# Scores of the two-headed tile moved ahead of the second head's transposes, and two copies exchanged between ScalarE and VectorE

## Chip, core and metric

The kernel runs on one core of a Trainium2 chip. The metric is the time of one execution on the device in microseconds (us); lower is better. The engines are TensorE (PE in the profile; PEld is its loading of weights), VectorE (DVE), ScalarE (ACT), GpSimd (POOL) and SyncE (SP), which issues most of the transfers.

## What is computed

Three stages in float32. The change touches only the first, the attention:

```python
def _attn_ref(q, k, v):                     # q, k, v: (4, 8, 1152, 64)
    B, H, S, D = q.shape
    scale = 1.0 / np.sqrt(D)
    q_pool = q.reshape(B, H, S // 2, 2, D).mean(axis=3)
    scores = scale * np.matmul(q_pool, k.transpose(0, 1, 3, 2))
    scores = scores - np.max(scores, axis=-1, keepdims=True)
    attn = np.exp(scores)
    attn = attn / (np.sum(attn, axis=-1, keepdims=True) + 1e-09)
    return np.matmul(attn, v)
```

The attention's output, as 2304 rows of 512, goes through a soft mixture of 8 experts (gating with `moe_phi`, two matrices of each expert) and then through `g = h - tanh(h)`, `g @ w_out`.

## The kernel before

**Pairs and rounds.** The 32 heads are done as 16 pairs. Each pair's 576 pooled queries are four tiles of 128 for each head and a rest of 64; the rests of both heads make one tile of 128 rows. So a pair has five rounds: r = 0, 1 (tiles 0 and 1, two heads each), r = 2, called MIX (one tile that holds 64 rows of either head), r = 3, 4 (tiles 2 and 3). Pairs 0, 1, 14 and 15 are written out, the other twelve run in a loop of two.

**A round.** TensorE multiplies q by K (`scores`, lines 256 and 259; q and K are held as a high and a low part, so three products) in three chunks of 512, 512 and 128 columns, into PSUM banks 0, 1, 2 for head 0 and 3, 4, 5 for head 1; MIX needs only banks 0 to 2. VectorE takes the row extreme: two reductions over the first chunks (L398), then one over the short chunk and both results (L402); for head 1 in one instruction over all 1152 columns (L410). ScalarE does the exponential of each head (L493, 1152 columns). TensorE transposes the nine 128x128 blocks of each head's probabilities (`turn_prob`, L290): head 0's chunks back into banks 0, 1, 2, head 1's into 6, 5, 4; for MIX in the order 2, 0, 1 into banks 0, 2, 1. They are copied to SBUF (`evac`): chunk 0 of both heads and chunk 1 of head 1 by ScalarE (L466), the others by VectorE (L372, for MIX L370). The product with V (`pv`, L306, bank 7) of what earlier rounds left is put between the scores and the transposes of rounds 3, 4, 0 and 1; MIX has none.

**The next pair's K and q.** In round MIX, TensorE also transposes the next pair's K (nine blocks, L239, banks 3 to 5, called `k_row`) and q (a rest block L247, then four blocks L242, bank 6 and the end of bank 5, `q_row`). VectorE copies K to `k_raw` (L448), ScalarE copies q to `q_raw` (L515), and GpSimd splits both into high and low parts (lines 208 to 214) for the next pair's round 0.

**What sets the order.** Everything is written out by hand: each engine runs its own list in program order and waits on semaphores. `first_evac` counts copied chunks 0, `second_a` and `second_b` chunk 1 of head 0 and of head 1, `third_evac` chunks 2. `banks_free` holds the waits of the scores for the banks. `first_evac`, `second_b` and `q_sum` are waited for ahead of the next pair's transposes, `k_copied` and `q_evac` ahead of round 3's scores, which overwrite `k_row` and `q_row`. The attention's output of the pair before is transposed (`turn_out`, L314 and L316) and scaled by VectorE (L427, L432) in rounds 1 and 3; `empty_v` (ScalarE) copies the V product out of bank 7.

After the last pair come the gating and the experts. The weights of experts 1 to 3 are loaded when marks in the last pair are reached, those of expert 4 when the gating ends, the later ones as slots come free.

Of the kernel before, what the change touches and what calls it, by code (L numbers as in the profile page):

```python
# [10 lines left out]
P = 128  # L11
# [6 lines left out]
def attention(nc, dram, sizes, sb, x, ident, rep, rep_ready, rep_step, early, prefetch):  # L18
# [38 lines left out]
    PV_EVAC_AT = {0: 0, 2: 1}  # L57

    with ExitStack() as ctx:
# [169 lines left out]
        def turned_as(r, c):  # L229

            return (1, 2, 0)[c] if r == MIX else c

        @block.tensor
        def _(pe):
            def turn_k_and_q(n, q_dst):

                pe.wait_ge(k_in, n * 32 + 32)
                for m in range(KT):
                    last = nc.tensor.transpose(k_row[:, m * P:(m + 1) * P], k_nat[:, m].rearrange("p h d -> p (h d)"), ident[:])  # L239
                last.then_inc(ktr_full, 1)  # L240
# [22 lines left out]
            def banks_free(p, r, c, first, last):  # L263

                before = tiles_of(p, r)
                if c == 0:
                    if r == MIX + 1:
                        wait(pe, third_evac, before)
                        if not last:
                            pe.wait_ge(k_copied, p + 1)  # L270
                    else:
                        wait(pe, first_evac, before - 1)
# [3 lines left out]
                elif r == MIX + 1:  # L276
                    wait(pe, first_evac, before)
                    if not last:
                        pe.wait_ge(q_evac, p + 1)
                elif r != MIX:  # L280
                    wait(pe, second_b, doubles_of(p, r))

            def turn_prob(p, r, h):
# [3 lines left out]
                for c in (2, 0, 1) if r == MIX else range(NCH):  # L287
# [32 lines left out]
            pe.wait_ge(ident_ready, 1)  # L320
            turn_q_rest(0, ps[:, TBANK, BANK - P:BANK])
            turn_k_and_q(0, first_q_row)

            def body(p, par, first, last):
                for r in range(ROUNDS):
                    for c in range(NCH):
                        banks_free(p, r, c, first, last)
                        if r == 0 and c == 0:
                            if first:
                                pe.wait_ge(first_kl, 1)  # L330
                                pe.wait_ge(first_ql, 1)
                            wait(pe, k_low, p)
                            wait(pe, q_low, p)
                        scores(p, par, r, c)

                    wait(pe, first_evac, tiles_of(p, r))
                    if r == MIX and not last:
                        wait(pe, second_b, doubles_of(p, r))
                        turn_q_rest(p + 1, ps[:, TBANK - 1, BANK - P:BANK])
                        turn_k_and_q(p + 1, q_row)  # L340
# [3 lines left out]
                    turn_prob(p, r, 0)  # L344
                    if r != MIX:
# [3 lines left out]
                if last:  # L349
# [4 lines left out]
                    turn_out(p, 1)  # L354

# [26 lines left out]
        def _(dve):  # L382
# [52 lines left out]
            def body(p, par, first, last):  # L435
                for r in range(ROUNDS):
                    tau = tiles_of(p, r)
                    minimum_by_chunks(p, r)
                    if r != MIX:
                        minimum_of_row(p, r)  # L440
# [4 lines left out]
                    if r == MIX and not last:  # L445
# [4 lines left out]
                    for c in (2, 1) if r == MIX else (1, 2):  # L450
                        dve.wait_ge(ptr_full, tau * NCH + turned_as(r, c) + 1)
# [12 lines left out]
        def _(act):  # L464
# [35 lines left out]
            def body(p, par, first, last):  # L500
                for r in range(ROUNDS):
                    tau = tiles_of(p, r)
                    if r in PV_EVAC_AT and not first:
                        empty_v(p - 1, PV_EVAC_AT[r])
# [3 lines left out]
                    act.wait_ge(ptr_full, tau * NCH + turned_as(r, 0) + 1)  # L508
                    evac(copy, r, 0, 0).then_inc(first_evac, 1)
                    if r == MIX:  # L510
                        if not last:
                            act.wait_ge(qtr_full, p + 2)
                            act.wait_ge(k_copied, p + 1)
                            wait(act, q_low, p)
                            nc.scalar.activation(q_raw[:], q_row, ACT.Copy, scale=EXP_SCALE).then_inc(q_evac, 1)  # L515
                    else:
                        act.wait_ge(ptr_full, tau * NCH + NCH + 1)
                        evac(copy, r, 1, 0).then_inc(first_evac, 1)
# [727 lines left out]
```

## Time and profile before

| | before |
|---|---|
| median of 3 runs | 886.7 us (885.58 to 887.46) |
| the profiled execution | 885.63 us, its span 883.8 us |
| mean granted TensorE clock | 0.984 of full |
| TensorE busy (PE / weight loads) | 811.5 us (92%) / 597.8 us (68%) |
| VectorE / ScalarE / GpSimd busy | 531.0 (60%) / 483.5 (55%) / 248.6 us (28%) |

The span of the profiled execution lies 1.8 us under its own time, and that time 1.1 us under the median. In the rows, times are microseconds from the span's start. A row such as "[0.68 <-ACT prob L493]" says how long the engine sat idle before it, and what released it. A matmul's row on PE has a modelled end, so starts are the safer reading.

### The profile page before, as it was taken

Reading aid. Unit: us, or ns where it says so; the run is one execution under the profiler, and the core shown is the slowest. Engines: PE = TensorE matmul, PEld = TensorE weight load, DVE = VectorE, ACT = ScalarE, POOL = GpSimd, SP = SyncE. Lnnn points to the kernel's source line nnn. Section 1 sums busy time; section 2 is a strip of 40 time slices with the busy share of each in tenths; the row PEclk is TensorE's granted clock in tenths of the full one; section 3 lists DMA queues with packets and bytes.
Section 4 is the critical chain, followed back from the end, with each engine's and each line's share of the span. In section 5 each row is a group of like instructions: output and inputs, shape, how many; then the busy total and the mean of one; then the engine's idle time right before and its main releaser. Section 6 shows DMA issues by size and latency. Waiting matters only on the chain. (4 is left out here: it accounts for less than half of the span.)

```text
span 883.8 us, 16411 instructions
## 1 busy us (share of the span) xinstructions
PE 811.5 (92%) x5819; PEld 597.8 (68%) x5819; DVE 531.0 (60%) x984; ACT 483.5 (55%) x729; POOL 248.6 (28%) x154
## 2 busy tenths in 40 slices
PE   3899999999999999999999988878678999999998
PEld 3676776776667677676677665634236888888886
DVE  2666666666666766766766754430037667677663
ACT  2566566566566566566566554220048666766672
POOL 2304304404404403403403300000038344334432
PEclk9999999999999999999999999979889999999999
DMA  5353303303303303303303164348960000000000
GB/s 134 131 145 81 81 2 82 80 1 80 80 0 80 80 0 80 80 0 80 80 0 80 63 252 162 125 170 315 404 253 1 25 24 24 24 24 24 24 24 24
DMA packets 82160, 75.49 MB, mean 85 GB/s; under 512 B 42448, under 2 KB 60880, under 8 KB 81616
## 3 DMA queue, kind: packets, MB, share of 16 engines
q1 hardware_dynamic: 79792, 74.47, 26.5%
q10 hardware_dynamic: 2336, 0.59, 0.3%
q8 instruction: 21, 0.34, 0.2%
q14 instruction: 11, 0.09, 0.0%
HBM read 70.32 MB, written 4.72 MB: 85 GB/s over the span
## 5 line engine op out<-in xcount | busy, mean ns | idle before, releaser
L493 ACT ACTIVATE prob<-ps,neg_max 128x1152 f32<-128x1152 f32 x144 | 175.7, 1221 | 186.6 <-DVE spare L402 186.6
L290 PE MATMUL ps<-ident,prob 128*128 128x128 f32 x1296 | 169.7, 280 | 29.3 <-ACT prob L493 27.1
L290 PEld LDWEIGHTS ps<-ident,prob 128*128 128x128 f32 x1296 | 140.7, 142 | 72.5 <-ACT prob L493 63.9
L306 PE MATMUL ps<-probT,v_nat 128*64 128x256 f32 (+1 forms) x1152 | 153.6, 411 | 0.0
L398 DVE TENSOR_REDUCE part_neg<-ps 128x1 f32<-128x512 f32 x160 | 109.7, 692 | 45.7 <-PE ps L259 38.2
L372 DVE COPY probT<-ps 128x128 f32<-128x128 f32 (+1 forms) x192 | 75.5, 421 | 99.5 <-PE ps L290 99.5
L466 ACT ACTIVATE probT<-ps 128x512 f32<-128x512 f32 x208 | 117.1, 594 | 32.1 <-PE ps L290 32.0
L208 POOL TENSOR_TENSOR kT<-k_raw,ones 128x1152 fp32r<-128x1152 f32 x15 | 31.6, 2107 | 311.0 <-DVE k_raw L448 311.0
L259 PE MATMUL ps<-kT,qT_hi 64*128 64x512 f32 (+1 forms) x768 | 112.2, 369 | 2.6 <-DVE qT_lo L389 2.6
L306 PEld LDWEIGHTS ps<-probT,v_nat 128*64 128x64 f32 x1152 | 77.3, 136 | 52.2 <-issue 5.7
L963 PE MATMUL ps<-w_hi,g_even 128*128 128x512 f32 x320 | 102.6, 392 | 2.2 <-POOL g_even L1047 2.0
L259 PEld LDWEIGHTS ps<-kT,qT_hi 64*128 64x128 f32 x768 | 68.1, 188 | 28.1 <-issue 10.6
L410 DVE TENSOR_SCALAR_CACHE_REDUCE spare<-ps 128x1152 f32<-128x1152 f32 x64 | 86.5, 1352 | 0.0
L963 PE MATMUL ps<-w_hi,g_odd 128*128 128x512 f32 x256 | 81.7, 390 | 0.0
L1021 ACT ACTIVATE slot<-ps 128x1024 f32<-128x1024 f32 x36 | 37.0, 1028 | 64.7 <-PE ps L947 64.6
L963 PEld LDWEIGHTS ps<-w_hi,g_even 128*128 128x128 f32 x320 | 60.1, 188 | 15.7 <-POOL g_even L1047 3.0
L259 PE MATMUL ps<-kT,qT_lo 64*128 64x512 f32 (+1 forms) x384 | 69.4, 355 | 0.0
L1086 DVE SCALAR_TENSOR_TENSOR slot<-slot,ps 128x1024 f32<-128x1024 f32 x36 | 44.0, 1222 | 38.6 <-ACT ps L1023 38.6
L1047 POOL TENSOR_TENSOR g_even<-slot,g_even 128x1024 fp32r<-128x1024 f32 x20 | 48.2, 2409 | 58.1 <-ACT g_even L1008 58.1
L1093 DVE COPY_PREDICATED slot<-slot,ps 128x1024 f32<-128x1024 uint32 x36 | 49.3, 1370 | 22.0 <-DVE slot L1086 20.3
L963 PE MATMUL ps<-w_lo,g_even 128*128 128x512 f32 x160 | 62.5, 391 | 0.0
L963 PEld LDWEIGHTS ps<-w_hi,g_odd 128*128 128x128 f32 x256 | 48.1, 188 | 9.7
(144 smaller groups left out, 1038.5 us busy)
## 6 DMA issues: line engine op xcount, KB each, us to landing
slot<-in_moe_w SPq DMA_DIRECT2D x16, 2048.0 KB, 12.8
v_nat<-in_v SPq DMA_DIRECT2D x16, 576.0 KB, 5.0
k_nat<-in_k SPq DMA_DIRECT2D x30, 288.0 KB, 4.0
q_nat<-in_q SPq DMA_DIRECT2D x32, 256.0 KB, 4.1
out<-res SPq DMA_DIRECT2D x18, 256.0 KB, 2.0
slot<-in_moe_w_in SPq DMA_DIRECT2D x2, 2048.0 KB, 20.8
slot<-in_moe_w_out SPq DMA_DIRECT2D x8, 512.0 KB, 16.7
q_nat_r<-in_q SPq DMA_DIRECT2D x32, 32.0 KB, 3.5
```

The costliest lines, as they stand in the source:

```text
L259: last = nc.tensor.matmul(ps[:, 3 * h + c, 0:k1 - k0], q[par][HALF[h], at], kT[par][HALF[h], part, k0:k1], start=(n == 0), stop=(n == 2))
L290: last = nc.tensor.transpose(dst[:, n * P:(n + 1) * P], prob[h][:, kt * P:(kt + 1) * P], ident[:])
L306: last = nc.tensor.matmul(ps[64 * h:64 * h + D, VBANK, 0:n], v_nat[par][:, h, kt, :], probT[g][:, kt, h, :], start=(kt == 0), stop=(kt == ...
L372: return copy(probT[g][:, k0:k1, h, col:col + P], src.rearrange("p (c q) -> p c q", c=n))
L398: nc.vector.tensor_reduce(part_neg[:, c:c + 1], ps[:, c, :], AX.X, ALU.min).then_inc(part_done, 1)
L410: nc.vector.tensor_scalar(spare[1][:], flat[:, 3 * BANK:3 * BANK + S], LARGE, LARGE, ALU.min, ALU.min, accum_out=neg_max[:, j:j + 1]).then ...
L466: return nc.scalar.activation(dst, src, ACT.Copy)
L493: nc.scalar.activation(prob[h][:], row, ACT.Exp, bias=neg_max[:, j:j + 1], scale=-1.0, accum_out=sums).then_inc(exp_done, 1)
L963: last = nc.tensor.matmul(ps[:, 2 * HB + i, :], a[par][:, ft * CW + i * P:ft * CW + (i + 1) * P], w(ft), start=(ft == 0 and k == 0), stop= ...
L1047: nc.gpsimd.tensor_tensor(g_block(g_lo, par, b), g[b % 2], g_block(g_hi, par, b).bitcast(F32), ALU.subtract).then_inc(gl_done, 1)
L1086: nc.vector.scalar_tensor_tensor(tv[b % 2], sq[b % 2], 1.0, h_of(b), ALU.subtract, ALU.mult).then_inc(series_done, 1)
L1093: nc.vector.copy_predicated(tv[b % 2], big[b % 2].bitcast(mybir.dt.uint32), th).then_inc(tanh_done, 1)
```

## The change

Five edits. (1) TensorE: MIX's scores are issued between round 1's transposes of head 0 and those of head 1. To free their banks in time, head 0 of round 1 is transposed in MIX's order and places (chunk 2 into bank 0, chunk 0 into bank 2, chunk 1 into bank 1). (2) TensorE: the next pair's K is transposed chunk by chunk, each chunk behind the wait for its bank, with q's rest between and q's other blocks last. (3) VectorE: MIX's reductions come between the copies of round 1's two heads; VectorE takes chunk 1 of head 1 of that round. (4) ScalarE: it copies K (and then q) right after MIX's exponential and ahead of MIX's chunk 0; `empty_v` of the second group moves to round 1, between its two copies. (5) At the start, K is transposed ahead of q's rest.

```diff
-    PV_EVAC_AT = {0: 0, 2: 1}
+    SHORT_FIRST = ((MIX - 1, 0), (MIX, 0))
...
-            place = (2, 1, 0) if r == MIX else ((0, 1, 2), (TBANK, 5, 4))[h]
+            place = (2, 1, 0) if (r, h) in SHORT_FIRST else ((0, 1, 2), (TBANK, 5, 4))[h]
...
+            def turn_next_k_and_q(p):
+
+                pe.wait_ge(k_in, (p + 1) * 32 + 32)
+                turn_k(0)
+                wait(pe, third_evac, tiles_of(p, MIX))
+                turn_k(1)
+                wait(pe, second_b, doubles_of(p, MIX))
+                turn_q_rest(p + 1, ps[:, TBANK - 1, BANK - P:BANK])
+                turn_k(2)
+                wait(pe, first_evac, tiles_of(p, MIX))
+                turn_q(q_row)
...
+                if r == MIX:
+                    if c == 0:
+                        pe.wait_ge(third_evac, before - 1)
+                    elif c == 1:
+                        pe.wait_ge(second_a, p * ROUNDS + r)
+                    else:
+                        pe.wait_ge(first_evac, before - 1)
...
+            pe.wait_ge(k_in, 32)
+            for c in range(NCH):
+                turn_k(c)
             turn_q_rest(0, ps[:, TBANK, BANK - P:BANK])
-            turn_k_and_q(0, first_q_row)
+            turn_q(first_q_row)
...
                     turn_prob(p, r, 0)
+                    if r == MIX - 1:
+                        all_scores(p, par, MIX, first, last)
                     if r != MIX:
...
-                    if r == MIX and not last:
-                        dve.wait_ge(ktr_full, p + 2)
-                        wait(dve, k_low, p)
-                        nc.vector.tensor_copy(k_raw[:], k_row).then_inc(k_copied, 1)
                     group_free(dve, p, r)
...
+                    if r == MIX - 1:
+                        minimum_by_chunks(p, MIX)
                     if r != MIX:
                         dve.wait_ge(ptr_full, tau * NCH + NCH + 3)
                         evac(nc.vector.tensor_copy, r, 1, 2).then_inc(third_evac, 1)
+                    if r == MIX - 1:
+                        dve.wait_ge(ptr_full, tau * NCH + NCH + 2)
+                        evac(nc.vector.tensor_copy, r, 1, 1).then_inc(second_b, 1)
...
+                    if r == MIX and not last:
+                        act.wait_ge(ktr_full, p + 2)
+                        wait(act, k_low, p)
+                        copy(k_raw[:], k_row).then_inc(k_copied, 1)
+                        act.wait_ge(qtr_full, p + 2)
+                        wait(act, q_low, p)
+                        nc.scalar.activation(q_raw[:], q_row, ACT.Copy, scale=EXP_SCALE).then_inc(q_evac, 1)
                     group_free(act, p, r)
...
                     evac(copy, r, 0, 0).then_inc(first_evac, 1)
...
+                    if r == MIX - 1 and not first:
+                        empty_v(p - 1, 1)
```

TensorE, pair 1, from the transposes of round 1's head 0 (`prob_79`; head 1 is `prob_80`) to MIX's; before:

```order
L290 MATMUL ps<-ident,prob_79 128x128 x9
L290 MATMUL ps<-ident,prob_80 128x128 x9
L256 MATMUL ps<-kT_74,qT_hi_76 128x512 x2
L256 MATMUL ps<-kT_74,qT_lo_78 128x512
L256 MATMUL ps<-kT_74,qT_hi_76 128x512 x2
L256 MATMUL ps<-kT_74,qT_lo_78 128x512
L256 MATMUL ps<-kT_74,qT_hi_76 128x128 x2
L256 MATMUL ps<-kT_74,qT_lo_78 128x128
L247 MATMUL ps<-ident,q_both_r 128x128
L239 MATMUL ps<-ident,k_nat 128x128 x9
L242 MATMUL ps<-ident,q_both 128x128 x4
L290 MATMUL ps<-ident,prob_79 128x128 x9
```

The same place in the changed kernel, up to q's last blocks:

```order
L312 MATMUL ps<-ident,prob_79 128x128 x9
L269 MATMUL ps<-kT_74,qT_hi_76 128x512 x2
L269 MATMUL ps<-kT_74,qT_lo_78 128x512
L269 MATMUL ps<-kT_74,qT_hi_76 128x512 x2
L269 MATMUL ps<-kT_74,qT_lo_78 128x512
L269 MATMUL ps<-kT_74,qT_hi_76 128x128 x2
L269 MATMUL ps<-kT_74,qT_lo_78 128x128
L312 MATMUL ps<-ident,prob_80 128x128 x9
L237 MATMUL ps<-ident,k_nat 128x128 x8
L248 MATMUL ps<-ident,q_both_r 128x128
L237 MATMUL ps<-ident,k_nat 128x128
L243 MATMUL ps<-ident,q_both 128x128 x4
```

The nine transposes of head 1 have moved from ahead of MIX's scores to behind them; the work is the same.

ScalarE, pair 1, rounds 1 and MIX; before:

```order
L466 ACTIVATE probT_81<-ps 128x4x128 x3
L466 ACTIVATE outT_86<-ps 128x256
L493 ACTIVATE prob_79,mix_sum_94<-ps,neg_max 128x1152
L466 ACTIVATE probT_81<-ps 128x8x64
L515 ACTIVATE q_raw<-ps 128x640
```

And in the changed kernel:

```order
L496 ACTIVATE probT_81<-ps 128x4x128
L496 ACTIVATE outT_86<-ps 128x256
L496 ACTIVATE probT_81<-ps 128x4x128
L523 ACTIVATE prob_79,mix_sum_94<-ps,neg_max 128x1152
L496 ACTIVATE k_raw<-ps 128x1152
L543 ACTIVATE q_raw<-ps 128x640
L496 ACTIVATE probT_81<-ps 128x8x64
```

One copy of round 1 is gone from ScalarE, and K's copy stands behind the exponential, ahead of q's and of MIX's own chunk 0.

## Rows read from the trace of the kernel before

**Rows 1.** Stretches: us, busy us (instructions) PE PEld DVE ACT POOL, PEclk, DMA, GB/s.

```profile
300.00:333.00 33.00, 31.50 (x257) 23.09 (x255) 22.34 (x48) 19.58 (x35) 9.31 (x7) 1.00 0.21 54
```

**Rows 2.** Waits, 35 to 500 us: who on whom, total us, times, longest.

```profile
POOL kT L208 <- DVE k_raw L448: 311.0, 15, 22.9
...
PEld ps L290 <- ACT prob L493: 56.9, 97, 1.2
```

**Rows 3.** Timeline, a pair in the loop: start us, us, engine, line, operation, [idle <-releaser].

```profile
324.28 0.97 PEld L290 LDWEIGHTS ps<-ident,prob 128*128 128x128 f32 x9 [0.68 <-ACT prob L493]
...
325.41 0.89 DVE L372 COPY probT<-ps 128x512 f32<-128x512 f32 x2 [0.90 <-PE ps L290]
325.48 0.96 PEld L290 LDWEIGHTS ps<-ident,prob 128*128 128x128 f32 x9 [0.23 <-ACT prob L493]
326.17 1.09 ACT L466 ACTIVATE probT<-ps 128x512 f32<-128x512 f32 x2 [0.26 <-PE ps L290]
326.41 0.30 PEld L256 LDWEIGHTS ps<-kT,qT_hi 128*128 128x128 f32 x2
...
327.13 0.30 PEld L256 LDWEIGHTS ps<-kT,qT_hi 128*128 128x128 f32 x2 [0.18 <-issue]
...
327.42 1.40 DVE L398 TENSOR_REDUCE part_neg<-ps 128x1 f32<-128x512 f32 x2 [0.41 <-PE ps L256]
...
328.18 0.14 PEld L247 LDWEIGHTS ps<-ident,q_both_r 128*128 128x128 f32 x1
...
328.96 0.41 DVE L402 TENSOR_SCALAR_CACHE_REDUCE spare<-ps,part_neg 128x128 f32<-128x128 f32 x1
...
329.53 1.36 DVE L448 COPY k_raw<-ps 128x1152 f32<-128x1152 f32 x1
329.57 1.22 ACT L493 ACTIVATE prob<-ps,neg_max 128x1152 f32<-128x1152 f32 x1 [2.04 <-DVE spare L402]
...
330.94 0.96 PEld L290 LDWEIGHTS ps<-ident,prob 128*128 128x128 f32 x9 [1.25 <-ACT prob L493]
...
331.74 0.60 ACT L466 ACTIVATE probT<-ps 128x512 f32<-128x512 f32 x1 [0.85 <-PE ps L290]
332.07 0.30 PEld L259 LDWEIGHTS ps<-kT,qT_hi 64*128 64x128 f32 x4 [0.17 <-issue]
...
332.18 0.69 DVE L370 COPY probT<-ps 128x512 f32<-128x512 f32 x1 [0.58 <-PE ps L290]
332.24 0.70 ACT L515 ACTIVATE q_raw<-ps 128x640 f32<-128x640 f32 x1
...
332.92 0.30 PEld L259 LDWEIGHTS ps<-kT,qT_hi 64*128 64x128 f32 x4 [0.32 <-DVE probT L370]
...
333.72 0.33 PE L259 MATMUL ps<-kT,qT_hi 64*128 64x128 f32 x4
```

**Rows 4.** The start: K's two loads, sizes and starts, and their times to landing.

```profile
L134 ACTq DMA_DIRECT2D k_nat<-in_k x2: 651/704/757, 0.7 to 1.4; - x2
...
DMA to landing us min/median/max: 5.0/5.5/6.0
```

**Rows 5.** The start: timeline, columns as in rows 3.

```profile
8.57 1.93 PEld L239 LDWEIGHTS ps<-ident,k_nat 128*128 128x128 f32 x9
...
10.94 1.13 ACT L466 ACTIVATE kT<-ps 128x1152 fp32r<-128x1152 f32 x1 [7.24 <-PE ps L239]
```

**Rows 6.** The last pair: timeline of PE, rounds 1 to 3.

```profile
521.06 1.20 PE L290 MATMUL ps<-ident,prob 128*128 128x128 f32 x9
...
527.75 1.54 PE L290 MATMUL ps<-ident,prob 128*128 128x128 f32 x9 [2.46 <-ACT prob L493]
...
531.90 0.34 PE L259 MATMUL ps<-kT,qT_hi 64*128 64x128 f32 x4
```

**Rows 7.** The last pair: one stretch, columns as in rows 1.

```profile
528.00:530.00 2.00, 2.00 (x13) 1.57 (x13) 0.97 (x2) 0.60 (x1) 0.00 (x0) 0.60 0.04 0
```

**Rows 8.** Transfers issued by SP after the attention: expert 4's first half.

```profile
585.48 0.37 SPq L1179 DMA_DIRECT2D slot<-in_moe_w  x1
```

More of the change, by code:

```diff
@@ L261, in scores, with banks_free @@
                 last.then_inc(scores_full, 1)
-            def banks_free(p, r, c, first, last):
+            def banks_free(p, r, c, last):
                 before = tiles_of(p, r)
-                if c == 0:
-                    if r == MIX + 1:
-                        wait(pe, third_evac, before)
+                if r == MIX:
[5 more added lines that the diff above has]
+                        pe.wait_ge(first_evac, before - 1)
+                elif r == MIX + 1:
+                    if c == 0:
+                        pe.wait_ge(third_evac, before)
                         if not last:
                             pe.wait_ge(k_copied, p + 1)
-                    else:
-                        wait(pe, first_evac, before - 1)
+                    elif c == 1:
+                        pe.wait_ge(second_a, p * ROUNDS + r)
+                    else:
+                        pe.wait_ge(first_evac, before)
+                        if not last:
+                            pe.wait_ge(q_evac, p + 1)
+                elif c == 0:
+                    wait(pe, first_evac, before - 1)
                 elif c == 1:
@@ L275, in banks_free @@
                     wait(pe, third_evac, before)
[L276 to L280, printed above, removed]
+                else:
                     wait(pe, second_b, doubles_of(p, r))
@@ L286, in turn_prob @@
                 pe.wait_ge(exp_done, tau + 1)
-                for c in (2, 0, 1) if r == MIX else range(NCH):
+                for c in (2, 0, 1) if (r, h) in SHORT_FIRST else range(NCH):
                     dst = turned(r, h, c)
@@ L320, in _ @@
             pe.wait_ge(ident_ready, 1)
+            pe.wait_ge(k_in, 32)
+            for c in range(NCH):
+                turn_k(c)
             turn_q_rest(0, ps[:, TBANK, BANK - P:BANK])
-            turn_k_and_q(0, first_q_row)
+            turn_q(first_q_row)
             def body(p, par, first, last):
                 for r in range(ROUNDS):
[L326 to L336, printed above, removed]
-                    if r == MIX and not last:
-                        wait(pe, second_b, doubles_of(p, r))
-                        turn_q_rest(p + 1, ps[:, TBANK - 1, BANK - P:BANK])
-                        turn_k_and_q(p + 1, q_row)
+                    if r != MIX:
+                        all_scores(p, par, r, first, last)
+                    if r != MIX:
+                        wait(pe, first_evac, tiles_of(p, r))
+                    elif not last:
+                        turn_next_k_and_q(p)
                     if r in OUT_AT and not first:
@@ L354, in body, with all_scores @@
                     turn_out(p, 1)
+            def all_scores(p, par, r, first, last):
+                for c in range(NCH):
+                    banks_free(p, r, c, last)
+                    if r == 0 and c == 0:
+                        if first:
+                            pe.wait_ge(first_kl, 1)
+                            pe.wait_ge(first_ql, 1)
+                        wait(pe, k_low, p)
+                        wait(pe, q_low, p)
+                    scores(p, par, r, c)
             def visit(p, par, r, first):
@@ L502, in body @@
                     tau = tiles_of(p, r)
[L503 to L504 removed]
+                    if r == 0 and not first:
+                        empty_v(p - 1, 0)
                     for h in range(heads_of(r)):
                         exponential(p, par, r, h)
+                    if r == MIX and not last:
[5 more added lines that the diff above has]
+                        nc.scalar.activation(q_raw[:], q_row, ACT.Copy, scale=EXP_SCALE).then_inc(q_evac, 1)
                     group_free(act, p, r)
[L508 removed]
+                    act.wait_ge(ptr_full, tau * NCH + turned_as(r, 0, 0) + 1)
                     evac(copy, r, 0, 0).then_inc(first_evac, 1)
[L510 to L516, printed above, removed]
+                    if r == MIX - 1 and not first:
+                        empty_v(p - 1, 1)
+                    if r != MIX:
                         act.wait_ge(ptr_full, tau * NCH + NCH + 1)
                         evac(copy, r, 1, 0).then_inc(first_evac, 1)
+                    if r != MIX and r != MIX - 1:
                         act.wait_ge(ptr_full, tau * NCH + NCH + 2)
```

20 lines of the change are left out of this document (10 added, 10 removed).

## Prediction

> **What bounds the kernel now.** I read the stretches first: in 33 us, the length of one pair, TensorE is busy 31.5 us at granted clock 1.00, VectorE 22.3, ScalarE 19.6 [rows 1]. So the attention goes at TensorE's pace, and what can be won is its idle time. The table of waits names it: the transposes' loads wait for the exponential 56.9 us in 97 places, while GpSimd waits for the copied K up to 22.9 us at a time, so it has much room [rows 2]. The timeline shows where a pair loses it. The largest hole is in round MIX: its transposes start at 330.94 after 1.25 us of idleness, because MIX has no V product to hide its chain (scores, reductions, L402, exponential) and the 14 transposes of the next K and q are too short a cover; 0.23 us more are lost in round 1, ahead of head 1's transposes at 325.48 [rows 3]. The rest of the kernel hangs on the end of the attention: the next weights are asked for at 585.48, when the gating ends [rows 8], so I take it that a shorter attention moves all of it forward unchanged.
>
> **The path through MIX, step by step.** I keep round 1's head 0 where it is (transposes start at 324.28) and put the changed order behind it, with durations from [rows 3].
>
> 1. Nine transposes take 0.97: MIX's scores of chunk 0 start at 325.25 instead of 326.41. Bank 0 is free by then, since the short chunk is transposed first and VectorE is idle.
> 2. Chunk 1 waits for bank 1, transposed last. In MIX before, VectorE's copy of a chunk 1 starts 1.24 after the first transpose (330.94 to 332.18), takes 0.69, and TensorE goes on 0.05 later (332.92). Here: 325.52, 326.21, 326.26. That is a new wait, some 0.5 us of TensorE, since chunk 0's scores take only 0.54 (0.72 from 326.41 to 327.13 less 0.18 idle). Behind it stand head 1's transposes and all of the next K.
> 3. Chunks 1 and 2 take 1.05 (327.13 to 328.18), so head 1's transposes start at 327.31 and end at 328.28. Their exponential is long done; the 0.23 goes.
> 4. The chain: the second reduction starts 0.99 after chunk 1's scores (327.42 plus 0.70, less 327.13), hence at 327.25, ends at 327.94; L402 0.14 later (328.96 after 328.82) at 328.08; exponential 0.61 later at 328.69; MIX's transposes could start 1.37 later (330.94 less 329.57), at 330.06.
> 5. Meanwhile TensorE: four blocks of K take 0.43 (at 0.108 each), to 328.71. Bank 4 needs VectorE's copy of head 1's chunk 2; VectorE is free at 328.49, the data are there at 327.31 plus 1.24, 328.55; chunks 2 and 1 together take 0.89 as at 325.41, the first 0.29 of it. So TensorE waits to 328.89, does four blocks to 329.32, waits for chunk 1 to 329.49 (new on VectorE, and the last thing on this path), does q's rest and K's last block to 329.70 and q's four blocks to 330.13.
> 6. MIX's transposes start at 330.13 (TensorE's own end, 0.07 behind the exponential) instead of 330.94: **0.81 us earlier**.
>
> **Does round 3 keep it?** Round 3's scores start 1.13 after MIX's transposes, at 331.26, and now need K copied by ScalarE. No row of the loop shows such a copy; the nearest is ScalarE's at the start, 1152 columns in 1.13 [rows 5], against VectorE's 1.36 [rows 3]. It needs K's last block (329.70 plus 0.27, as 1.24 less 0.97) and the end of the exponential (1.30 after its start, 1.22 and a short read-out, 329.99): it ends at 331.12, and TensorE sees it at 331.17. So it is hidden by only 0.09, and by 0.32 more that TensorE then spends waiting for chunk 1 anyway [rows 3]. Then come q's copy (0.70) and MIX's chunk 0 (0.60), done by about 332.4; the scores of chunk 2, which wait for both, come at 333.72 less 0.81, 332.91. Cover 0.5. VectorE loses the K copy of 1.36 and gains a copy of 0.69 in a place where it was idle. `empty_v` fits between two copies of ScalarE. GpSimd gets K some 0.2 us later against this frame and waited over 20 us for it [rows 2]. SP's load of the next K waits for K's transposes, 0.2 us later in the frame, and has a whole pair.
>
> So 15 pairs (the last turns no K) at 0.8 give **12.0 us**. What no row shows is how much each new wait on TensorE costs beyond its semaphore; from 0 to the 0.18 idle ahead of 327.13 each [rows 3], three of them: 0 to 0.5 a pair. I take near 0, since that idle is explained by the copy it waits for. The other bound is the exponential's, 0.88 a pair.
>
> **The last pair.** No K and q: the exponential decides. Round 1's head 0 starts at 521.06, MIX's transposes at 527.75, 6.69 later [rows 6]. By step 4 they start 5.78 later (330.06 less 324.28): **0.9 us**. Behind its idle time of 2.46 the granted clock is 0.60 over 528 to 530 [rows 7], a mix of the 1.2 and 2.4 GHz levels, and from MIX's transposes to round 3's chunk 2 it takes 4.15 [rows 6] where it takes 2.78 in the loop (330.94 to 333.72) [rows 3]. So the low clock costs 1.4. The new idle time there is about 1.8; holes of 1.25 do not bring the clock down. I take half, **0.7**, with 0 and 1.4 as ends.
>
> **The start.** K's second load is issued at 1.4 and lands 6.0 later, at 7.4 [rows 4]; its transposes start at 8.57, behind q's rest [rows 5]. So up to 1.1 is won. But TensorE works there at its low level (1.93 for nine blocks, against 0.97), and if the rise to 2.4 GHz does not move along, about half is given back. I take **0.7**, between 0.5 and 1.1. The Trainium skill, "TensorE: Matmul & The Clock Gate", Part 1 (The HAM clock gate), says that the gate's observation runs freely and does not start with the kernel's work. By that the half is the likelier value; no row here shows it.
>
> **Sum.** 12.0 + 0.9 + 0.7 + 0.7 = 14.3 us. Against the profiled execution, 885.6 becomes 871.3; its time lies 1.1 under the median, so against the median of the runs, 886.7 becomes **872.4**.
>
> **Rivals.**
>
> *A. ScalarE decides round 3.* The K copy has 0.09 us of cover, and everything in front of it (head 1's chunk 1 on VectorE, K's last block) can only be later than I have it. If the three new waits cost half their bound and K's copy comes late by the same, 0.4 a pair is kept: 6.0 + 0.9 + 0.5, and the time is **879.3**. For it: two handovers of 0.05 each are all the slack there is. Against: TensorE's own path is as long. Chance 0.15.
>
> *B. More than forecast.* The exponential's bound in every pair (13.2), the whole start (1.1), the last pair at the high clock (2.3): 16.6, **870.1**. Chance 0.10.
>
> *C. The clock falls in MIX.* After the change, from the end of MIX's scores (327.31) to round 3's (331.26) TensorE does only transposes, with small holes, for 3.95 us; before it was 3.89 (328.18 to 332.07), 1.25 of it idle, and the clock stayed at 1.00 [rows 1, 3]. If it fell, each fall would cost 1.4 as in the last pair; it decides from about 9 of the 15 pairs, where it eats the 12.0. In all 15, with only the start's 0.5 kept: 15 times (1.4 less 0.8) is 9.0, and the time is **895.2**. The Trainium skill, "TensorE: Matmul & The Clock Gate", Part 4 (PE-mode transpose), says of transposes that they do not count as TensorE being busy in the same way. By that rule this is the result; the trace speaks against it, since the loop's holes between scores were nearly as long and never brought the clock down. Chance 0.04.
>
> *D. Nothing is gained in the loop*, because MIX's hole moves whole into the new waits of steps 2 and 5 (0.5 + 0.2 + 0.2 against 1.25 + 0.23, so they would have to be 0.6 longer). Left is the start: **886.0**. Chance 0.03.
>
> **Numbers.** The forecast has 0.68, A 0.15, B 0.10, C 0.04, D 0.03. The forecast's own range, with 0.6 to 0.88 a pair and the ends of the other terms, is 870 to 876; with B and most of A it is 869.5 to 879.5. About 0.2% (1.8 us) is what a measurement of this kernel can tell from no change: faster 0.93, same 0.03, slower 0.04.
>
> **What would show it.** Right: MIX's transposes start 5.8 to 6.0 us after head 0's of round 1 (6.66 before); a wait of TensorE of about 0.5 on VectorE's copy ahead of MIX's chunk 1; K's copy on ScalarE about 1.13 long, with little or no wait of round 3 on it; the pair's period 32.1 instead of 32.9. A shows as idle time ahead of round 3's scores, released by ScalarE. C shows as granted clock under 1.00 between 36 and 500 us. I am wrong if round 3's own waits grow by what MIX loses, or if a later stage starts earlier but ends as before.

## The result

The changed kernel takes 875.95 us (median of 4 runs, 873.17 to 876.39) against 886.14 before (4 runs), 0.9879 of it (95% interval 0.9852 to 0.9906): 10.2 us faster, where 14.3 were forecast. The profiled execution took 876.1, its span is 874.3, 9.5 under the span before.

The profile after, first the stretch of 32 us that answers to [rows 1], columns as there; then the waits of TensorE from 35 to 490 us, to be set beside [rows 2]:

```profile
323.00:355.00 32.00, 31.52 (x253) 22.90 (x253) 21.68 (x48) 20.05 (x35) 9.20 (x6) 1.00 0.22 55
```

```profile
POOL kT L208 <- ACT k_raw L496: 315.2, 15, 22.8
...
PEld ps L312 <- ACT prob L523: 36.2, 72, 1.0
...
PEld ps L269 <- DVE probT L401: 7.3, 14, 0.5
...
PEld ps L272 <- DVE probT L399: 4.8, 15, 0.3
...
PEld ps L248 <- issue: 3.0, 12, 0.3
PEld ps L237 <- DVE probT L401: 2.6, 14, 0.2
```

The same 31.5 us of work now fit into 32 us, and the transposes wait for the exponential 20 us less. The new waits are small: MIX's chunk 1 on VectorE's copy (L269, 0.5 a pair), K's second chunk (L237, 0.2) and q's rest (L248, 0.3). The row on L272 is the wait that [rows 3] has ahead of 332.92, and it has kept its size. No wait of TensorE on ScalarE's copy of K is there.

The timeline of one pair in the loop, to be read beside [rows 3]:

```profile
317.63 0.96 PEld L312 LDWEIGHTS ps<-ident,prob 128*128 128x128 f32 x9 [0.59 <-ACT prob L523]
...
318.56 0.30 PEld L269 LDWEIGHTS ps<-kT,qT_hi 128*128 128x128 f32 x2
...
319.61 0.30 PEld L269 LDWEIGHTS ps<-kT,qT_hi 128*128 128x128 f32 x2 [0.52 <-DVE probT L401]
...
320.66 0.96 PEld L312 LDWEIGHTS ps<-ident,prob 128*128 128x128 f32 x9
...
321.44 0.41 DVE L431 TENSOR_SCALAR_CACHE_REDUCE spare<-ps,part_neg 128x128 f32<-128x128 f32 x1
...
322.06 1.22 ACT L523 ACTIVATE prob<-ps,neg_max 128x1152 f32<-128x1152 f32 x1
322.25 0.42 PEld L237 LDWEIGHTS ps<-ident,k_nat 128*128 128x128 f32 x4 [0.18 <-DVE probT L401]
322.92 0.14 PEld L248 LDWEIGHTS ps<-ident,q_both_r 128*128 128x128 f32 x1 [0.25 <-issue]
...
323.39 1.13 ACT L496 ACTIVATE k_raw<-ps 128x1152 f32<-128x1152 f32 x1
323.52 1.01 PEld L312 LDWEIGHTS ps<-ident,prob 128*128 128x128 f32 x9
...
324.71 0.30 PEld L272 LDWEIGHTS ps<-kT,qT_hi 64*128 64x128 f32 x4 [0.17 <-issue]
```

Counted from the first transpose of round 1's head 0 (324.28 before, 317.63 now):

| start of | before | forecast | measured |
|---|---|---|---|
| MIX's scores, chunk 0 | 2.13 | 0.97 | 0.93 |
| MIX's scores, chunk 1 | 2.85 | 1.98 | 1.98 |
| head 1's transposes | 1.20 | 3.03 | 3.03 |
| MIX's exponential | 5.29 | 4.41 | 4.43 |
| ScalarE's copy of K | | 5.71 | 5.76 |
| MIX's transposes | 6.66 | 5.85 | 5.89 |
| round 3's scores | 7.79 | 6.98 | 7.08 |

GpSimd's first operation on K, the same line in both kernels, gives the period of a pair: its 15 starts, before and after.

```profile
L208 POOL TENSOR_TENSOR kT<-k_raw,ones x15: 2107/2107/2111, 34.8 to 495.3; 128x1152 fp32r<-128x1152 f32 x15
```

```profile
L208 POOL TENSOR_TENSOR kT<-k_raw,ones x15: 2106/2107/2109, 35.5 to 484.9; 128x1152 fp32r<-128x1152 f32 x15
```

Divided by 14 these are 32.89 and 32.10: 0.79 a pair, 11.1 in the 14 periods. But the first start has become later, and what the end shows is less than 11.1. So the time has to be followed by marks. The table has them for all kernels of this study, each from one profiled execution, in us from the span's start: where TensorE starts its first scores, the scores of round 3 in the first pair, the gating's first transposes and the experts' first matmuls. The period is worked out from L208 as above.

| kernel | first scores | round 3, first pair | period | gating starts | experts start | span |
|---|---|---|---|---|---|---|
| before | 14.3 | 35.7 | 32.89 | 551.8 | 592.5 | 883.8 |
| after | 13.0 | 35.6 | 32.10 | 538.3 | 582.9 | 874.3 |
| e1_old_start | 14.6 | 35.4 | 32.09 | 538.0 | 582.6 | 873.8 |
| e2_start_only | 13.1 | 34.4 | 32.90 | 550.4 | 591.1 | 882.3 |
| e3_k_on_vector | 13.2 | 35.3 | 32.21 | 539.0 | 579.2 | 870.3 |
| e4_chunk_on_scalar | 13.2 | 33.9 | 32.22 | 538.5 | 581.5 | 872.4 |
| e5_order_round1 | 13.0 | 32.4 | 31.74 | 529.7 | 570.0 | 861.0 |
| e6_order_both | 13.1 | 34.8 | 31.59 | 529.9 | 574.7 | 866.1 |
| e7_busy_start | 13.7 | 32.1 | 32.10 | 534.7 | 579.9 | 871.2 |
| e8_busy_end | 13.4 | 35.5 | 32.10 | 539.6 | 579.8 | 870.8 |
| e9_all | 12.1 | 29.9 | 31.58 | 526.3 | 567.4 | 858.9 |
| e10_delay_end | 13.1 | 32.8 | 32.10 | 536.4 | 583.2 | 875.1 |
| e11_order_busy_end | 13.1 | 33.6 | 31.59 | 530.0 | 570.6 | 861.7 |
| e12_transposes_end | 13.1 | 35.4 | 32.10 | 539.3 | 579.7 | 870.9 |

Before and after compared: 1.3 ahead at the first scores, 0.1 at round 3 of the first pair, 13.5 when the gating starts, 9.6 when the experts start, 9.5 at the end. So 1.2 us of the start and the whole gain of the first pair are lost in the first 36 us, and 3.9 us in the gating. From the experts' start to the end both take the same (291.3 and 291.4). Both stretches that lose time have one thing in common. The granted clock of TensorE there, in stretches with the columns of [rows 1]; first the changed kernel:

```profile
14.00:18.00 4.00, 1.94 (x14) 1.67 (x10) 3.08 (x6) 1.28 (x3) 0.29 (x1) 0.50 0.88 258
18.00:24.00 6.00, 5.92 (x28) 5.23 (x30) 1.31 (x4) 3.02 (x6) 1.39 (x2) 0.51 0.01 6
27.00:31.00 4.00, 3.64 (x14) 3.29 (x15) 1.23 (x5) 2.09 (x5) 0.00 (x0) 0.57 0.00 0
```

```profile
539.00:549.00 10.00, 10.00 (x55) 6.78 (x58) 3.03 (x4) 2.60 (x4) 0.80 (x1) 0.52 0.72 269
```

and the gating's first 4 us in the kernel before:

```profile
551.80:555.80 4.00, 3.96 (x25) 2.74 (x25) 1.42 (x3) 1.30 (x2) 1.55 (x1) 1.00 1.03 399
```

0.50 is the 1.2 GHz level, 1.00 the 2.4 GHz one. How much this costs is seen on the gating's 80 transposes, before and then after:

```profile
L605 PE MATMUL ps<-ident,x x80: 271/272/330, 551.8 to 567.7; 128*128 128x128 f32 x64, 64*128 64x64 f32 x16
```

```profile
L639 PE MATMUL ps<-ident,x x80: 271/328/473, 538.3 to 558.1; 128*128 128x128 f32 x64, 64*128 64x64 f32 x16
```

From the first to the last start it is 15.9 us before and 19.8 after, which is the whole 3.9.

### The profile page after: what moved, and what is told of

Same layout as the page of the kernel before. It is cut to its first block and busy times, and to the rows that moved or that the text cites. A ratio compares the mean times of both kernels' runs of the same rounds, so it can differ in the third digit from the quotient of the medians.

```text
span 874.3 us, 16359 instructions
## 1 busy us (share of the span) xinstructions
PE 818.6 (94%) x5819; PEld 601.0 (69%) x5819; DVE 521.7 (60%) x985; ACT 490.9 (56%) x728; POOL 248.5 (28%) x154
## 5 line engine op out<-in xcount | busy, mean ns | idle before, releaser
L401 DVE COPY probT<-ps 128x128 f32<-128x128 f32 (+1 forms) x208 | 86.6, 442 | 90.3 <-PE ps L312 89.0
L496 ACT ACTIVATE probT<-ps 128x512 f32<-128x512 f32 x192 | 109.2, 594 | 44.7 <-PE ps L312 44.7
L208 POOL TENSOR_TENSOR kT<-k_raw,ones 128x1152 fp32r<-128x1152 f32 x15 | 31.6, 2107 | 315.2 <-ACT k_raw L496 315.2
L272 PE MATMUL ps<-kT,qT_hi 64*128 64x512 f32 (+1 forms) x768 | 111.5, 367 | 2.5 <-DVE qT_lo L418 2.5
L272 PEld LDWEIGHTS ps<-kT,qT_hi 64*128 64x128 f32 x768 | 67.5, 187 | 28.0 <-issue 10.4
L272 PE MATMUL ps<-kT,qT_lo 64*128 64x512 f32 (+1 forms) x384 | 69.3, 354 | 0.0
```

The lines of the kernel that those rows point to most:

```text
L272: last = nc.tensor.matmul(ps[:, 3 * h + c, 0:k1 - k0], q[par][HALF[h], at], kT[par][HALF[h], part, k0:k1], start=(n == 0), stop=(n == 2))
L401: return copy(probT[g][:, k0:k1, h, col:col + P], src.rearrange("p (c q) -> p c q", c=n))
L496: return nc.scalar.activation(dst, src, ACT.Copy)
```

## The experiments

The theory to test: (one) the loop gains what the steps say, and TensorE's clock takes back 4 us in the gating and a good part of the start. The rival: (two) the clock is a companion only, and the lost time has another cause, such as the weights' transfers, which run at about 400 GB/s beside the gating's first transposes, or the new start. A third (three): the clock is the cause, but whether it falls is decided by where in time the stretch lies, and not by the idle time ahead of it (the expectations of e10 and e11 call this one theory two). And of the parts of the change: what is the exchange of copies worth, and is the new wait of 0.52 on the path?

Each ratio below is to runs of the kernel before that were made beside the experiment; their median was 885.7 to 887.9. The changed kernel was not run again beside the experiments, so a difference from its 875.95 of one or two microseconds says little.

### The start undone, and the start alone

```diff
+            turn_q_rest(0, ps[:, TBANK, BANK - P:BANK])
             pe.wait_ge(k_in, 32)
             for c in range(NCH):
                 turn_k(c)
-            turn_q_rest(0, ps[:, TBANK, BANK - P:BANK])
             turn_q(first_q_row)
```

> The changed kernel with the start undone: q's rest is transposed ahead of K again. The two traces show the changed kernel 1.3 us ahead at the first scores and only 0.1 us ahead at round 3 of the first pair, with granted clock 0.50 from about 14 to 24 us; so theory one (the clock takes back what the start wins): this kernel is at the same point of the first pair within 0.5 us and its time is within 1.5 us of the changed kernel's 876.0. Theory two (the start's gain is kept and something else is late): it is slower by 1.1, about 877. Both expect the pair's period of 32.10 us.

Measured: 875.99 us (4 runs, 875.6 to 877.53), 0.9891 of before (0.9874 to 0.9909). At round 3 of the first pair it is 0.2 ahead of the changed kernel, though its first scores come 1.6 later. Undoing the edit costs nothing that can be measured.

The same lines exchanged the other way round in the kernel before:

> The kernel before with nothing but the new start. By my prediction 0.5 to 1.1 us faster, about 885.5. Theory one (the clock takes it back): between 884.5 and 887.5, with first scores 1.3 us earlier and round 3 of the first pair less than 0.5 us earlier. The pair's period stays 32.89 us.

Measured: 887.3 us, 1.0023 of before (1.0001 to 1.0045); its 10 runs spread from 884.15 to 893.36, with mean granted clocks of 0.984 and 0.969 at these two ends. Its profiled execution, the fastest of the ten, is 1.3 us ahead at round 3 of the first pair, where theory one had allowed less than 0.5, and 1.5 at the end (882.3 against 883.8). So the start won 1.3 us in this execution, and over the runs it wins nothing. Its value is not settled by this; that it isn't a sure 0.7 is.

### The exchange of copies undone, one at a time

K copied by VectorE again:

```diff
+                    if r == MIX and not last:
+                        dve.wait_ge(ktr_full, p + 2)
+                        wait(dve, k_low, p)
+                        nc.vector.tensor_copy(k_raw[:], k_row).then_inc(k_copied, 1)
                     group_free(dve, p, r)
...
                     if r == MIX and not last:
-                        act.wait_ge(ktr_full, p + 2)
-                        wait(act, k_low, p)
-                        copy(k_raw[:], k_row).then_inc(k_copied, 1)
+                        act.wait_ge(k_copied, p + 1)
```

> The changed kernel with K copied by VectorE again (ahead of MIX's own copies), ScalarE copying q behind it. My reading of the path: the copy takes 1.36 and starts when K's last block is there, so it ends about 0.2 us later than on ScalarE, and MIX's chunks 2 and 1 stand behind it on VectorE: round 3's chunk 0 is held some 0.4 us and its chunk 1 some 0.2 more, 0.4 to 0.6 us a pair, 6 to 9 us in all: 882 to 885. Rival (the exchange of engines is worth nothing, the order of the scores is all): within 1.5 us of 876.

Measured: 871.32 us (4 runs, 870.33 to 872.88), 0.9832 (0.9811 to 0.9853): *faster* than the changed kernel, against both expectations. The table tells how: the period is 32.21, so the loop is slower, by 0.11 a pair or 1.5 us. But from the gating's start to the experts it takes 40.2 us instead of 44.6; the clock did not fall there:

```profile
539.00:549.00 10.00, 9.81 (x92) 7.14 (x93) 3.56 (x7) 3.26 (x5) 1.57 (x1) 1.00 0.80 301
```

92 operations in the same ten microseconds in which the changed kernel did 55. The holes of TensorE ahead of the gating are as in the changed kernel, and the gating starts only 0.8 later. The loop's part was also less than I had expected (0.11, not 0.4 to 0.6). Its timeline, at the start of round 3:

```profile
323.58 1.36 DVE L477 COPY k_raw<-ps 128x1152 f32<-128x1152 f32 x1 [0.60 <-PE ps L237]
...
325.19 0.30 PEld L272 LDWEIGHTS ps<-kT,qT_hi 64*128 64x128 f32 x4 [0.47 <-DVE probT L399]
...
325.79 0.40 PEld L272 LDWEIGHTS ps<-kT,qT_hi 64*128 64x128 f32 x4
```

Round 3's chunk 0 waits 0.47 for MIX's chunk 2 behind K's copy, but the wait of 0.32 that chunk 1 had is gone in return. I had added the two; the one stands in the place of the other.

Chunk 1 of head 1 copied by ScalarE again:

```diff
-                    if r == MIX - 1:
-                        dve.wait_ge(ptr_full, tau * NCH + NCH + 2)
-                        evac(nc.vector.tensor_copy, r, 1, 1).then_inc(second_b, 1)
...
-                    if r != MIX and r != MIX - 1:
+                    if r != MIX:
```

> The changed kernel with chunk 1 of round 1's head 1 copied by ScalarE again. The transposes of that chunk are done about 0.5 us after chunk 0's, so ScalarE would start this copy at about the time at which MIX's exponential starts now, and the exponential goes behind it: 0.35 to 0.45 us later, MIX's transposes 0.3 us later, 15 pairs: 4.5 us, about 880.5. Rival (TensorE has its own work there and hides it): within 1.5 us of 876.

Measured: 873.37 us (4 runs, 870.02 to 877.79), 0.9857 (0.9814 to 0.99). The period is 32.22: 0.12 a pair is what this half of the exchange is worth, not 0.3. The exponential is late as expected, and the wait shows on MIX's transposes:

```profile
322.88 0.96 PEld L312 LDWEIGHTS ps<-ident,prob 128*128 128x128 f32 x9 [0.38 <-ACT prob L520]
```

but the wait ahead of q's rest (0.25) is gone, which gives most of it back. The total again says nothing on this part: in its profile the start is 1.7 ahead at round 3 of the first pair and the gating 1.6 shorter than in the changed kernel. The gating started here at the high level too (its first 40 transposes take 6.75) and lost its time later. A second stretch of low clock lies in the gating of every kernel, where TensorE waits several times for 1.0 to 1.2 us; in the changed kernel it is this one:

```profile
566.00:573.00 7.00, 4.77 (x25) 1.46 (x29) 5.99 (x10) 1.38 (x3) 0.00 (x0) 0.55 0.01 2
```

In e4 it runs from about 561 to 571.5, at 0.50, and the clock falls once more at 574.5.

So the halves of the exchange are worth 0.11 and 0.12 a pair, each undone by itself; whether they add was not tried. What is left of the 0.79 belongs to the other edits together: the place of MIX's scores, the order of round 1's chunks, K's transposes chunk by chunk, and the place of `empty_v`. No run separates these.

### The new wait ahead of MIX's chunk 1

Head 0 of round 1 transposed in the order 2, 1, 0, so that bank 1 is not the last (the function that gives each chunk's place in the count is changed to match, here and in the next kernel):

```diff
-                for c in (2, 0, 1) if (r, h) in SHORT_FIRST else range(NCH):
+                for c in (2, 1, 0) if (r, h) == (MIX - 1, 0) else (2, 0, 1) if (r, h) in SHORT_FIRST else range(NCH):
```

> The changed kernel, but head 0 of round 1 is transposed in the order 2, 1, 0 instead of 2, 0, 1, so that bank 1, for which MIX's chunk 1 waits 0.52 us in the changed kernel, can be emptied four transposes (0.43 us) earlier. If that new wait is on the path, MIX's chain and so its transposes come 0.3 to 0.4 us earlier in each pair: 5 to 6 us, about 870.5. Rival (the wait is covered by the later waits for K's banks or by K's copy): 876.

Measured: 864.52 us (4 runs, 862.83 to 865.24), 0.973 (0.9677 to 0.9782), and the period is 31.74:

```profile
L208 POOL TENSOR_TENSOR kT<-k_raw,ones x15: 2107/2107/2108, 32.3 to 476.7; 128x1152 fp32r<-128x1152 f32 x15
```

0.36 a pair, as expected: the wait that the change introduced was on the path, and 5 us were to be had by another order of the same transposes. Its profile is 13.3 shorter than the changed kernel's. Beside the 5.0 of the loop that is mostly the start (round 3 of the first pair at 32.4, 3.2 earlier) and a gating of 40.3 us, 4.3 shorter, with the same holes ahead of it.

The order 2, 1, 0 in MIX too:

```diff
-                for c in (2, 0, 1) if (r, h) in SHORT_FIRST else range(NCH):
+                for c in (2, 1, 0) if (r, h) in SHORT_FIRST else range(NCH):
```

> The same order 2, 1, 0 in round 1 and in MIX. In MIX it takes away round 3's wait of 0.32 us ahead of its chunk 1, unless K's or q's copy on ScalarE, or MIX's chunk 0 behind them, then comes last: 0.2 to 0.3 us a pair more than the order in round 1 alone, about 867. Rival (ScalarE's row of copies decides round 3's chunk 2): as with round 1 alone, and a wait of round 3 on ScalarE shows.

Measured: 865.42 us, 0.9723 (0.9658 to 0.9787), with runs of 861.11 and 862.9 (mean clock 0.988 and 0.980) and of 867.93 and 868.42 (0.976 and 0.974). The period is 31.59, 0.15 less again. The wait of 0.32 has gone, of which half arrives. In its profile the clock falls at the gating's start, which lasts 44.8 us; so the kernel with the better loop has the worse median, though the ranges of the two overlap.

### Work in the waits

The functions of the kernel stay, and TensorE multiplies the identity with itself where it would wait; nobody reads the results. At the start (20 while K is loaded, 12 ahead of the first scores, 12 each in rounds 0 and 1 of the first pair):

```diff
+            def fill(bank, n):
+                for _ in range(n):
+                    nc.tensor.matmul(ps[:, bank, 0:P], ident[:], ident[:], start=True, stop=True)
...
+            fill(0, 20)
             pe.wait_ge(k_in, 32)
...
             turn_q(first_q_row)
+            fill(0, 12)
...
+                    if first and r < 2:
+                        fill(7, 12)
                     visit(p, par, r, first)
```

> The changed kernel with matmuls of the identity, whose results nobody reads, in four waits of TensorE at the start: 20 while K is loaded, 12 ahead of the first scores, 12 each in rounds 0 and 1 of the first pair. Theory one (the low clock costs the start its gain and more): the granted clock is 1.00 by the first scores and stays, round 3 of the first pair starts 2.5 to 5 us earlier than at 35.59, and the time falls by as much, to about 872. Theory two (the clock has no part in it): 876 or a little more, as added work can only delay.

Measured: 873.03 us (4 runs, 871.85 to 874.89), 0.9825 (0.977 to 0.988). Round 3 of the first pair starts at 32.1 instead of 35.6, although the fills were too long: K's transposes start 1.7 later than they could. By itself this shows little: e10 and e5, without fills at the start, reach that point at 32.8 and 32.4. What the fills at the start are worth is shown by e9 below.

And at the end of the attention, in the three waits ahead of the gating:

```diff
                 if last:
+                    fill(3, 7)
                     wait(pe, first_evac, tiles_of(p, ROUNDS))
                     turn_out(p, 0)
                     pv(p, par, 1, 0, len(PV_ORDER))
+                    fill(3, 4)
                     pe.wait_ge(out_evac, p * 2 + 1)
                     turn_out(p, 1)
+                    fill(3, 6)
```

> The changed kernel with such matmuls in the three waits of TensorE at the end of the attention (7, 4 and 6). In the changed kernel's trace the gating starts 13.5 us earlier than before, and its first 25 us are 3.9 us longer, with granted clock 0.50 from 539.3 to 549.7. Theory one (that is the clock, and the waits ahead of it bring it down): clock 1.00 there, and 2 to 4 us faster, about 873. Theory two (the stretch is slow for another reason, such as the weights' transfers that run beside it): no change of the 8.4 us that its first transposes take, 876.

Measured: 870.84 us (4 runs, 869.7 to 872.57), 0.9794 (0.9741 to 0.9847): 5.1 under the changed kernel's median, all four runs below all of its. The gating starts 1.3 later and takes 40.2 instead of 44.6:

```profile
539.00:549.00 10.00, 9.32 (x90) 6.75 (x89) 3.55 (x7) 3.00 (x5) 1.81 (x1) 1.00 0.70 262
```

The transfers beside it are the same (share 0.70 against 0.72), so they are not what slowed it. But the fills also move the gating in time, to where e3, without any fills, kept the high level as well (539.0). So this alone doesn't tell whether it is their work that counts. For that the gating was held back without work for TensorE, by two copies on ScalarE:

```diff
                     empty_v(p, 0)
                     empty_v(p, 1)
+                    act.wait_ge(ptr_full, PAIRS * TILES * NCH)
+                    copy(prob[0][:], flat[:, 0:S])
+                    copy(prob[1][:], flat[:, 0:S])
```

> The changed kernel with two copies of 1152 columns, whose results nobody reads, on ScalarE at the end of the attention, which hold the gating back by 1.0 to 1.5 us while TensorE stays idle. It puts the gating's start where the kernel with the fills had it (539.6, against 538.3), without their work. Theory one (the fills' work held the clock): the granted clock falls to 0.50 again for about 10 us and the gating is as long as in the changed kernel or longer, 44.6 us from its first transposes to the experts; time about 877. Theory two (it is only a matter of where in time the stretch falls, which the fills moved by 1.3 us): no fall, 40.2 us, time about 873.

Measured: 877.12 us (4 runs, 874.05 to 877.79), 0.9884 (0.9856 to 0.9911). Its timeline at the gating's start, then the stretch:

```profile
536.38 10.48 PE L642 MATMUL ps<-ident,x 128*128 128x128 f32 x40 [2.01 <-DVE unit L739]
```

```profile
537.00:547.00 10.00, 10.00 (x41) 6.64 (x44) 2.37 (x4) 2.60 (x4) 0.92 (x1) 0.50 0.63 234
```

The first 40 transposes take 10.5 us, which took 6.75 before, and the way to the experts 46.8. But its start ran 2.8 us faster, so the gating began at 536.4 and not at the 539.6 aimed at: this run doesn't separate idle time from place in time. Its runs overlap with the changed kernel's, too. A better pair is e6 and e11 below, the same loop without and with the fills, whose gatings start at 529.9 and 530.0.

Over all profiled executions it stands like this. In the four kernels with fills ahead of the gating (e8, e9, e11, e12) the clock was 1.00 at its start each time. Of the nine without fills and without e10's delay, which all have the same three holes, it fell in four (the changed one at 538.3, e1 at 538.0, e6 at 529.9, e7 at 534.7) and stayed in five (before, e2, e3 at 539.0, e4 at 538.5, e5 at 529.7). So the holes don't bring the clock down every time. That filling them prevents the fall is what the runs speak for, theory one; with four executions it is not shown beyond theory three.

Transposes in the place of the matmuls (14, 8 and 12):

```diff
-                    nc.tensor.matmul(ps[:, bank, 0:P], ident[:], ident[:], start=True, stop=True)
+                    nc.tensor.transpose(ps[:, bank, 0:P], ident[:], ident[:])
```

> The changed kernel with transposes of the identity in place of the matmuls in the three waits at the attention's end (14, 8 and 12, about the same time). If transposes hold the clock as matmuls do: no fall at the gating's start, about 870.8 as with matmuls. If they don't: the fall is back, 44.6 us from the gating's first transposes to the experts, about 877.

Measured: 872.21 us (4 runs, 870.12 to 872.71), 0.9829 (0.9805 to 0.9853), gating 40.4 us:

```profile
539.00:549.00 10.00, 9.52 (x90) 6.88 (x90) 3.54 (x7) 3.25 (x5) 1.80 (x1) 1.00 0.72 272
```

With transposes in the holes the clock didn't fall either, and the median is 1.4 above that with matmuls, with overlapping ranges. The Trainium skill, "TensorE: Matmul & The Clock Gate", Part 4 (PE-mode transpose), has it that they don't count as work in the same way; by that this kernel would have been at 877, and the measurement speaks against it. So does the kernel before, where TensorE did 40 transposes in a row from 551.8, for 6.7 us, at 1.00. It is not the whole story: in the changed kernel the clock, once down, stayed down while TensorE did the same 40 transposes, for 9.9 us, and came back at about 549.6, 1.5 us into the matmuls behind them; in the later stretch it was back at 573.5, 4.5 us after TensorE had started on matmuls (568.97). Whether transposes bring the clock back as matmuls do was not tried.

### Together

The order 2, 1, 0 in both places with the fills at the end:

> Order 2, 1, 0 in both places with the fills at the attention's end alone. The kernel with that order had the low clock from 531.3 to 541.5 and 44.8 us from the gating's first transposes to the experts. Theory one (the fills hold the clock): no fall there, 40.2 us, about 1.3 us later start: about 862.5 against 865.4. Theory two (a matter of place in time): either is possible; with a fall, 867.

Measured: 863.7 us (4 runs, 863.53 to 864.09), 0.9742 (0.9721 to 0.9764), gating 40.6 us. The spread of its runs is 0.6 us, where the same order without the fills (e6) had 7.3: two of e6's runs, at 861.1 and 862.9, were faster than these, and two, at 867.9 and 868.4, slower.

And with shorter fills at the start as well (13, 11, 10 and 10):

> Order 2, 1, 0 in both places, with the matmuls nobody reads at the start (13, 11, 10 and 10) and at the end of the attention (7, 4, 6). From the traces so far: round 3 of the first pair at about 31.5 (32.08 with the longer fills), 14 periods of 31.59, no low clock at the gating's start: gating at about 527.5, experts 40.2 later, end of the span about 858.5, time about 860. If the fills don't hold the clock, 4 us more, 864.

Measured: **859.97 us** (5 runs, 859.07 to 860.67), 0.9697 of before (0.9678 to 0.9716). Round 3 of the first pair starts at 29.9, the period is 31.58, the gating 41.1. It beats both kernels, and its runs lie within 1.6 us. All of them are below all of e11's, from which it differs by the fills at the start alone; so these are worth 3.7 us, and 29.9 is a point of the first pair that no kernel without them reached before 32.4.

## Why the prediction was right, and where it was off

The direction held, and the range of 870 to 876, this one with some luck: 875.95 is at its very end, and it is there because a loss that the prediction did not have (3.9) was partly made up by a last pair that won more than forecast. The size was 10.2 and not 14.3. By its own steps:

- **The path through MIX** (steps 1 to 6). Right in every step, to 0.1 us; the table in the result has them side by side. The wait of 0.5 ahead of chunk 1 came as worked out, and e5 shows that it was on the path.
- **Round 3 keeps it.** Right: ScalarE's copy of K takes 1.13, as the row at the start had it, and no wait of TensorE on it shows. That it had to be ScalarE is worth 0.11 a pair (e3).
- **The loop, 12.0.** Measured 11.1 in 14 periods, for which 11.2 was forecast; the first pair's share was lost with the start.
- **The last pair, 0.9 and 0.7.** Too low. Its rows, beside [rows 6]:

```profile
509.81 1.20 PE L312 MATMUL ps<-ident,prob 128*128 128x128 f32 x9
...
515.41 1.20 PE L312 MATMUL ps<-ident,prob 128*128 128x128 f32 x9 [1.37 <-ACT prob L523]
...
518.20 0.33 PE L272 MATMUL ps<-kT,qT_hi 64*128 64x128 f32 x4
```

  MIX's transposes come 5.60 after head 0's (5.78 forecast, 6.69 before), and 2.79 later is chunk 2 of round 3, so the low clock is gone there: 1.1 and 1.4.
- **The start, 0.7.** Off. It won 1.3 at the first scores and 0.1 at round 3 of the first pair, in place of 1.5 (0.7, and the first pair's 0.8). The half that the clock gives back was right up to round 1's transposes, which start 0.7 earlier (28.07 and 27.36). What I did not have is that the clock could fall again there, behind 2.48 us of idle time; in the kernel before, behind the same idle time, it did not:

```profile
28.07 2.39 PE L290 MATMUL ps<-ident,prob 128*128 128x128 f32 x18 [2.48 <-ACT prob L493]
```

```profile
27.36 2.15 PE L312 MATMUL ps<-ident,prob 128*128 128x128 f32 x9 [2.48 <-ACT prob L523]
```

  18 transposes in 2.39 before, nine in 2.15 after.
- **"A shorter attention moves all of it forward unchanged."** This is the step that failed. I checked that the transfers move along, which they do (experts to end 291.3 and 291.4), and put the clock at nothing, although the holes of 1.05, 0.57 and 1.08 us of TensorE ahead of the gating are in the trace of before. Of the 13.5 us won by then, 3.9 were lost in the gating, all of it by the low clock over its 80 transposes and the matmuls among them. What brought the clock down there in this kernel and not in the one before stays open: with work in those holes (e8) the gating takes 40.2 and with more idle time (e10) 46.8, but e3 takes 40.2 with the holes as they are.
- **The rivals.** A fell (no wait on K's copy), D fell (the period). C was placed in MIX, where nothing fell: the clock is 1.00 in the loop. The clock did take time back, but at the start and in the gating, and nothing shows that C's reason, transposes that don't count, was at work.

Added up: 11.1 + 0.1 + 2.5, less 0.2 in small things, is 13.5 at the gating; less 3.9 and 0.1 it is 9.5 in the two profiled spans, and 10.2 between the medians.

## What to carry to other kernels

A stage with no filler work is best covered by pulling its first operations ahead of the work before it; then read which chunk the pulled work needs first, and produce that one first (here 5 us for one changed order of three chunks). Where TensorE's clock can fall, compare kernels by the period of the loop and by marks along the profile, not by the total alone: two kernels here (e3 and e4) had a slower loop than the changed kernel and a better median, by what the clock did outside of it (in e4 with overlapping ranges). And try work in the holes of TensorE at the start and ahead of a dense stretch: at the start it won 3.7 us (e9 against e11), ahead of the gating the four kernels with it never had the low clock at its start.

## What the runs showed of the hardware that I had not expected

- Four kernels have the same program for TensorE up to the last pair (the changed one, e8, e10, e12), and their round 3 of the first pair starts at 35.6, 35.5, 32.8 and 35.4. What the clock does at the start differs from one execution to the next, by 2.8 us in these four. That fits what the Trainium skill, "TensorE: Matmul & The Clock Gate", Part 1 (The HAM clock gate), says of an observation that runs freely.
- Ahead of some 10 us at 0.50 no hole was longer than 1.08 us: 1.05, 0.57 and 1.08 us of idle time around 4 us of V products and five short transposes. Why the kernel before, e2, e3, e4 and e5, with the same holes, kept 1.00 there was not settled.
- A granted clock of 1.00 at the start doesn't mean the high level. In the kernel with the old start the stretch of 18 to 24 us reads 1.00, and its 18 transposes take 3.83 us, where 2.2 is usual:

```profile
18.00:24.00 6.00, 3.85 (x22) 3.63 (x20) 2.84 (x7) 3.74 (x7) 1.68 (x2) 1.00 0.19 72
```

```profile
20.21 3.83 PE L312 MATMUL ps<-ident,prob 128*128 128x128 f32 x18 [2.15 <-ACT prob L523]
```

  There the durations, not the granted clock, tell the level.
